# Loading k and v over all 128 partitions, and keeping attention's output in SBUF until its stores

## The chip, the cores and the metric

One core of one Trainium2 chip runs the whole program. The time is device microseconds of one execution. The profile is one further execution, recorded by the hardware profiler; its span is counted from the first to the last instruction of the program.

## The reference

Three stages follow one another. The first is an attention with 32 memory slots for each of 64 heads, the second a dense layer with a sigmoid gate, the third a layer of eight experts with one expert for each token.

```
q, k, v: (8, 8, 576, 64)   phi: (8, 8, 576, 32)
a    = softmax(phi, over the 32 slots)
k_m  = a^T k ;  v_m = a^T v                     # per head: 32 x 64
x    = softmax(q k_m^T / 8) v_m                 # per head: 576 x 64
x    -> (4608 tokens, 512)
h    = x @ w_in (512 x 2048) ; x2 = (h * sigmoid(1.702 h)) @ w_out (2048 x 512)
out  = gate * relu(x2 @ w1[e]) @ w2[e]          # e = the token's best of 8 experts
```

## The kernel before

**Attention.** The 64 heads are worked in 16 groups of four (`NG` = 16, numbered 0 to 15). For a group, SP loads phi (288 KB, `load_phi`), k and v (576 KB each) and q (576 KB, both in `load_qkv`) into one of two buffers, so the loads of group g+2 are issued when group g has released its buffer: `s_phT` for phi, `s_kv` for k and v, `s_qtr` for q. All of these DMAs stand in SP's queue in that order. k takes two DMAs, and so does v: one for heads 0 and 1 on partitions 0 to 63, one for heads 2 and 3 on partitions 64 to 127. The source of each is written with its 64 rows first and the two heads second.

On the compute side VectorE turns phi round (`phi_in`, L1101 and L1103), ScalarE takes its exponential, TensorE transposes it (L619), sums k and v (L631), transposes q (L605) and computes the scores (L649). VectorE does most of the softmax of the group before (L1113 to L1138), and the output matmuls of the group before that are in `out_half` (L590). Each engine goes through its steps in one fixed order. `groups` writes groups 0 to 2 out, runs groups 3 to 14 as three rounds of a loop over four groups, and writes group 15 out.

ScalarE copies the output of a group from PSUM to `xo` (`x_out`, L884), which has two buffers, and stores the group at once (L887) into the DRAM tensor `xT_dram`, on ScalarE's own DMA queue.

**Dense layer.** It runs over nine tiles of 512 tokens. The x of a tile is loaded from `xT_dram` (`load_x`); the first tile needs the tokens of groups 0 and 1 only, the second those of groups 0 to 3. The first load of x is the last but two of SP's DMAs before the tiles. `x_hi` and `x_lo` split x in two float32r parts on ScalarE and VectorE inside the last group, and TensorE starts tile 0 with `mm1(0, 0)` (L672) between the last steps of attention. `mm1` and `mm2` (L706) alternate from there, sixteen of each in a tile, 12 matmuls each.

**Weights.** `W` holds w_in in its first half and w_out in its second, each value as a high and a low part. The first four chunks of w_in are loaded during groups 0 to 3. The other 28 are loaded by SP (`load_w`) and split by GpSimd (`split_w`, L1515 and L1517; `split_w_in`, L1525 and L1527) during tile 0, beginning when the x of tile 0 has been split. `mm1(0, f)` for f = 4, 8, 12 and every `mm2(0, f)` wait for those splits. `stage_a_done` is a wait for all stores of x; it stands on ScalarE and VectorE in step 2 of tile 0 and on SP behind the last load of weights.

**Experts.** The last stage starts from tables that the earlier tiles build; its block loop is not touched. Two constants, `blk8` and `load8`, are loaded between the dense layer and the experts (L527), each from one row of DRAM to one partition.

Of the kernel before, what the change touches and what calls it, by code (L numbers as in the profile page):

```python
# [31 lines left out]
P = 128  # L32
B, H, S, D, M = 8, 8, 576, 64, 32
HG = 4
# [57 lines left out]
def build(nc, q, k, v, phi, w_in, w_out, w_gate, w_ogate, w1, w2, cst, out):  # L92
# [15 lines left out]
    with ExitStack() as ctx:  # L108
# [5 lines left out]

        SLOT = 4 * EW
# [4 lines left out]
        sb("to_512", [P, 96 - RING * (NE + 4)])  # L120
        W = sb("W", [P, 2 * SLOT], F32R)
# [16 lines left out]
        with ExitStack() as a:  # L138
# [25 lines left out]
            xo = sbt(a, "xo", [P, 2, 2, S])  # L164
# [86 lines left out]
        s_xst = [sem(f"xT_stored{i}") for i in range(2)]  # L251
# [63 lines left out]

        def stage_a_done(eng):

            for i in range(2):
                eng.wait_ge(s_xst[i], 16 * B)
# [32 lines left out]
        def groups(eng, body):  # L352
# [3 lines left out]
            with eng.Fori(0, (NG - 4) // 4) as m:  # L356
                for j in range(4):
                    body(4 * m + (3 + j), 2 * m + (3 + j) // 2, (3 + j) % 4)
            body(NG - 1, B - 1, 3)
# [49 lines left out]
        def _(sp):  # L409
# [10 lines left out]
            def load_qkv(g, b, u):  # L420

                wait(sp, s_kv, g - 1)
                for w, src in enumerate((k_v, v_v)):
                    for hh in range(2):
                        heads = src[bass.ds(g * HG + 2 * hh, 2)].rearrange("h (p c) d -> p h (c d)", c=CA)
                        sp.dma_start(kvm[u][hh * PA:(hh + 1) * PA, w], heads).then_inc(s_kvl[u], 16)  # L426
# [42 lines left out]
            with sp.Fori(0, (NG - 8) // 4) as m:  # L469
                for j in range(4):  # L470
                    sp_group(4 * m + (3 + j), 2 * m + (3 + j) // 2, (3 + j) % 4)
            for g in range(NG - 5, NG - 2):
                sp_group(g, g // 2, g % 4)

            for i in range(2):
                sp.wait_ge(s_xst[i], 16)
            load_x(0)
# [19 lines left out]
            def sp_tile(t, first=False, last=False):  # L497
# [3 lines left out]
                if first:  # L501
                    for k in range(1, 4):
# [5 lines left out]
                        if k == 1:  # L508
                            load_x(t + 1)
# [336 lines left out]
        def _(act):  # L846
# [32 lines left out]
            def x_out(g, b, u, i, bank=4):  # L879
# [17 lines left out]
            def group(g, b, r):  # L897
# [14 lines left out]
                if not isinstance(g, int) or g >= 2:  # L912
                    x_out(g - 2, b - 1, u, 0)
# [4 lines left out]
                if not isinstance(g, int) or g >= 2:  # L918
                    x_out(g - 2, b - 1, u, 1)
# [3 lines left out]
            x_out(NG - 2, B - 1, 0, 0)  # L923
# [720 lines left out]
```

## Time and profile before

| what | value |
|---|---|
| median of 3 runs | 1402.93 us (1402.65 to 1410.83) |
| profiled execution, its own time | 1402.57 us |
| its span | 1400.9 us |
| attention, up to the first `mm1` | 153.1 us |
| TensorE busy, whole span | 1351.8 us (96%) |
| TensorE busy, 60 to 80 us | 16.94 of 20 us |
| TensorE busy, 180 to 200 us | 20.00 of 20 us |

The profiled execution's time and its span differ by 1.7 us, which lie around the span. Where the engines are busy all the time a stage is bound by them; where one waits, the row of its wait names what came last. The DMA share is the mean busy share of the 16 DMA engines; it can be over 1, since packets overlap.

### The profile page before, as it was taken

The numbers are of one execution on the slowest core, as the hardware profiler recorded it, in microseconds if no ns is written. First come the engines' busy times: TensorE is split into PE (matmuls) and PEld (weight loads), VectorE is DVE, ScalarE is ACT, GpSimd is POOL, SyncE is SP. The second block draws the span as 40 slices with busy tenths as digits, with TensorE's granted clock in tenths as the row PEclk, the third lists the DMA queues.
The fourth block names the chain that finished last, engine by engine and source line by source line (L and its number), as shares of the span: only waits on it lengthen the run. The fifth ranks groups of instructions, "written<-read, shape, count | busy, mean of one in ns | idle before, by whom it ended". The sixth has DMA issues, their size and how long they took to land.

```text
span 1400.9 us, 26210 instructions
## 1 busy us (share of the span) xinstructions
PE 1351.8 (96%) x7922; PEld 1094.9 (78%) x7923; DVE 681.5 (49%) x1400; ACT 403.2 (29%) x725; POOL 517.7 (37%) x612
## 2 busy tenths in 40 slices
PE   5888899999999999999999999999999999999997
PEld 4566688888888888888888888887788888888885
DVE  4789633344353343433534344436655555555553
ACT  2455422222232232222322223223332222223221
POOL 1100486345443343433433334331434333433331
PEclk9999999999999999999999999999999999999999
DMA  9999635656556556465465654665784688649882
GB/s 229 290 325 313 234 100 168 194 200 194 181 191 183 179 169 182 171 187 175 160 183 176 179 192 147 184 189 203 236 257 119 164 254 249 185 115 261 246 237 61
DMA packets 164843, 275.31 MB, mean 197 GB/s; under 512 B 20179, under 2 KB 57316, under 8 KB 164788
## 3 DMA queue, kind: packets, MB, share of 16 engines
q1 hardware_dynamic: 104260, 197.16, 44.7%
q10 hardware_dynamic: 47408, 45.63, 12.7%
q0 software_dynamic: 13120, 31.82, 7.3%
q8 instruction: 31, 0.51, 0.2%
q14 instruction: 24, 0.20, 0.0%
HBM read 146.03 MB, written 100.45 MB: 176 GB/s over the span
## 4 chain that ended last, share of the span: by engine, by line
PE 86%; DVE 5%; DMA 3%; issue 3%; SPq 2%; ACT 0%; ACTq 0%; POOL 0%; DVEq 0%; POOLq 0%
PE ps L672 28%; PE ps L706 28%; PE ps L776 14%; PE ps L747 14%; DMA ph<-in_phi 1%; PE ps L716 1%; DMA qraw<-in_q 1%; SPq L426 1%; SPq L454 1%; PE ps L649 1%; DVE cmeta L1123 1%; DVE phT L1101 1%; DMA cq<-ch 1%; PE ps L631 0%; DMA cmeta<-record_scratch 0%
## 5 line engine op out<-in xcount | busy, mean ns | idle before, releaser
L672 PE MATMUL ps<-xs,W 128*128 (+1 forms) x1728 | 417.6, 391 | 1.1 <-DVE xs L1162 1.1
L706 PE MATMUL ps<-W,gs 128*128 128x512 f32 x1728 | 415.3, 390 | 0.1
L672 PEld LDWEIGHTS ps<-xs,W 128*128 128x128 f32 x1728 | 323.1, 188 | 72.0 <-issue 4.1
L706 PEld LDWEIGHTS ps<-W,gs 128*128 128x128 f32 x1728 | 324.3, 188 | 68.1 <-DVE gs L1217 0.8
L1215 DVE TENSOR_TENSOR gate<-ps,gate 128x512 f32<-128x512 f32 x144 | 99.6, 691 | 364.0 <-ACT gate L932 363.7
L932 ACT ACTIVATE gate<-ps 128x512 f32<-128x512 f32 x144 | 86.2, 598 | 471.3 <-PE ps L672 470.8
L776 PE MATMUL ps<-W,chT 128*128 (+1 forms) x936 | 218.3, 390 | 1.2 <-DVE chT L1348 1.2
L747 PE MATMUL ps<-W,cx 128*128 (+1 forms) x936 | 218.5, 390 | 0.5 <-issue 0.5
L1540 POOL CAST whi<-raw 128x512 fp32r<-128x512 f32 x128 | 81.3, 635 | 337.9 <-DMA raw<-in_moe_w 337.9
L776 PEld LDWEIGHTS ps<-W,chT 128*128 128x128 f32 x936 | 175.6, 188 | 38.3 <-issue 2.0
L747 PEld LDWEIGHTS ps<-W,cx 128*128 128x128 f32 x936 | 175.6, 188 | 37.3 <-issue 1.1
L1542 POOL TENSOR_TENSOR raw<-raw,whi 128x512 f32<-128x512 f32 x128 | 172.3, 1346 | 21.5 <-POOL whi L1540 20.0
L1217 DVE TENSOR_TENSOR gs<-gate,gs 128x512 fp32r<-128x512 f32 x144 | 120.4, 836 | 99.0 <-ACT gs L936 99.0
L340 POOL DMA_DIRECT2D crec<-record_scratch x160 | 90.0, 562 | 192.1 <-DMA out<-cy,cmeta 114.6
L936 ACT CAST gs<-gate 128x512 fp32r<-128x512 f32 x144 | 89.4, 621 | 115.1 <-DVE gate L1215 113.2
L997 ACT CAST chT<-cqT 128x512 fp32r<-128x512 f32 x41 | 25.2, 620 | 201.4 <-issue 159.8
L1348 DVE TENSOR_TENSOR chT<-cqT,chT 128x512 fp32r<-128x512 f32 x78 | 53.1, 691 | 38.9 <-ACT chT L997 37.6
L1312 DVE TENSOR_TENSOR cx<-cxT,cx 128x512 fp32r<-128x512 f32 x40 | 43.7, 1092 | 57.4 <-ACT cx L965 57.4
L1548 POOL DMA_INDIRECT record_scratch<-rec,posi x36 | 36.3, 1008 | 94.1 <-DVE posi L1277 85.7
L1597 POOL DMA_INDIRECT out<-cy,cmeta x39 | 43.1, 1106 | 70.5 <-ACT cy L1005 62.8
L1326 DVE TENSOR_SCALAR ch<-ps 128x512 f32<-128x512 f32 x37 | 25.5, 691 | 66.5 <-PE ps L747 66.3
L1335 DVE STREAM_TRANSPOSE cqT<-cq 128x512 f32<-128x512 f32 x78 | 50.6, 687 | 13.2 <-DMA cq<-ch 11.4
(158 smaller groups left out, 891.1 us busy)
## 6 DMA issues: line engine op xcount, KB each, us to landing
W<-expert_scratch SPq DMA_DIRECT2D x24, 2048.0 KB, 11.7
raw<-in_moe_w SPq DMA_DIRECT2D x128, 256.0 KB, 2.8
expert_scratch<-whi SPq DMA_DIRECT2D x128, 256.0 KB, 2.6
expert_scratch<-raw SPq DMA_DIRECT2D x128, 256.0 KB, 2.9
cq<-ch ACTq DMA_DIRECT2D x156, 128.0 KB, 3.9
crec<-record_scratch POOLq DMA_DIRECT2D x160, 64.0 KB, 5.6
kvm<-in_k SPq DMA_DIRECT2D x32, 288.0 KB, 5.2
kvm<-in_v SPq DMA_DIRECT2D x32, 288.0 KB, 7.0
```

The costliest lines, as they stand in the source:

```text
L340: eng.dma_start(crec[b * M:(b + 1) * M, r % 3], rows[:, b * P:(b + 1) * P].rearrange("(h n) d -> n h d", n=M)).then_inc(loaded, 16)
L672: mm = pe.matmul(ps[:, f % 2, :], W[:, col:col + P], xs[:, bass.ds(x0 + (x_lo * K1 + c) * T, T)], start=(c == 0 and w_lo + x_lo == 0), sto ...
L706: mm = pe.matmul(ps[:, 2 + s, :], gs[:, f % 2, g_lo, s * P:(s + 1) * P], W[:, col:col + DM], start=(f == 0 and g_lo + w_lo == 0), stop=(f ...
L747: mm = pe.matmul(ps[:, 3 * u + j, :], cx[:, u, x_lo, c, :], W[:, bass.ds(col, 512)], start=(c == 0 and x_lo + w_lo == 0), stop=(c == K1 - ...
L776: mm = pe.matmul(ps[:, 5 + r % 2, :], chT[:, r % 2, h_lo, c, :], W[:, bass.ds(col, DM)], start=(c == 0 and h_lo + w_lo == 0), stop=(c == C ...
L932: act.activation(gate[:, f % 2, :], ps[:, f % 2, :], ACT.Sigmoid, scale=QTOK).then_inc(b_sig, 1)
L936: act.copy(gs[:, f % 2, 0, :], gate[:, f % 2, :]).then_inc(b_ghi, 1)
L1215: dve.tensor_tensor(gate[:, f % 2, :], ps[:, f % 2, :], gate[:, f % 2, :], ALU.mult).then_inc(b_g, 1)
L1217: dve.tensor_tensor(gs[:, f % 2, 1, :], gate[:, f % 2, :], gs[:, f % 2, 0, :].bitcast(F32), ALU.subtract).then_inc(b_glo, 1)
L1348: dve.tensor_tensor(by_h(1, j), cqT[:, j * 512:(j + 1) * 512].rearrange("p (h c n) -> p h c n", h=2, n=M), by_h(0, j).bitcast(F32), ALU.su ...
L1540: pool.tensor_copy(whi[:, u, :], raw[:, u, :]).then_inc(e_hi, 1)
L1542: pool.tensor_tensor(raw[:, u, :], raw[:, u, :], whi[:, u, :].bitcast(F32), ALU.subtract).then_inc(e_lo, 1)
```

## The change

The change has two parts. First, the two DMAs for k (and the two for v) are cut the other way: each covers all 128 partitions and one head of each pair, and its source is written with the pair (2) first and the 64 rows second. Each still moves 288 KB in 128 runs of 2304 bytes.

Second, the copied output of every group stays in SBUF, in `xk`, a region that lies under the part of `W` that the later chunks of weights are split into. The stores are issued in five sets, by different engines: groups 0 and 1 by SP before the loads of group 13, with a wait for them and the first load of x before the loads of group 15; groups 8 and 7 by SP behind all loads; groups 6 and 5 by ScalarE in group 14, groups 4, 3 and 2 in group 15; groups 13, 12, 14, 15 in step 1 of tile 0, and 11, 10, 9 in step 2. GpSimd waits for the stores whose place in `W` it is about to write. The loop over groups now runs twice, and groups 11 to 15 are written out. The wait for all stores moves to ScalarE's step 15 of tile 0 and is gone from VectorE.

```diff
+        STORES = ((0, 1), (8, 7), (6, 5, 4, 3, 2), (13, 12, 14, 15), (11, 10, 9))
...
+            sbt(a, "before_xk", [P, SLOT // 2])
+            xk = sbt(a, "xk", [P, NG * 2 * S])
         W = sb("W", [P, 2 * SLOT], F32R)
...
-            xo = sbt(a, "xo", [P, 2, 2, S])
...
+        def kept(g):
+            return xk[:, bass.ds((NG - 1 - g) * 2 * S, 2 * S)].rearrange("p (a n) -> p a n", a=2)
+        def store_x(eng, i, groups):
+            for g in groups:
+                eng.dma_start(xT_dram[2 * (g % 2) * P:(2 * (g % 2) + 2) * P, g // 2 * S:(g // 2 + 1) * S].rearrange("(a p) n -> p a n", a=2),
+                              kept(g)).then_inc(s_xst[i], 16)
+        def stored_x(eng, i):
+            eng.wait_ge(s_xst[i], 16 * len(STORES[i]))
...
-            with eng.Fori(0, (NG - 4) // 4) as m:
+            with eng.Fori(0, (NG - 8) // 4) as m:
...
-            body(NG - 1, B - 1, 3)
+            for g in range(NG - 5, NG):
+                body(g, g // 2, g % 4)
...
                 for w, src in enumerate((k_v, v_v)):
-                    for hh in range(2):
-                        heads = src[bass.ds(g * HG + 2 * hh, 2)].rearrange("h (p c) d -> p h (c d)", c=CA)
-                        sp.dma_start(kvm[u][hh * PA:(hh + 1) * PA, w], heads).then_inc(s_kvl[u], 16)
+                    heads = src[bass.ds(g * HG, HG)].rearrange("(a h) (p c) d -> h a p (c d)", a=2, c=CA)
+                    for h2 in range(2):
+                        sp.dma_start(kvm[u][:, w, h2], heads[h2]).then_inc(s_kvl[u], 16)
...
+            sp.wait_ge(s_xo, 2 * 2)
+            store_x(sp, 0, STORES[0])
             for g in range(NG - 5, NG - 2):
                 sp_group(g, g // 2, g % 4)
-            for i in range(2):
-                sp.wait_ge(s_xst[i], 16)
-            load_x(0)
+                if g == NG - 4:
+                    stored_x(sp, 0)
+                    load_x(0)
+            sp.wait_ge(s_xo, 2 * 9)
+            store_x(sp, 1, STORES[1])
             load_w(K1, w_out_v[0])
...
                         if k == 1:
+                            stored_x(sp, 2)
                             load_x(t + 1)
...
-                if i == 0:
-                    wait(act, s_xst[u], 16 * b)
-                act.copy(xo[:, u, :, i * HS:(i + 1) * HS], ps[:, bank:bank + 2, 0:HS]).then_inc(s_xo, 1)
-                if i == 1:
-                    wait(act, s_xo, 2 * g + 2)
-                    act.dma_start(xT_dram[2 * u * P:(2 * u + 2) * P, bass.ds(b * S, S)].rearrange("(a p) n -> p a n", a=2),
-                                  xo[:, u]).then_inc(s_xst[u], 16)
+                act.copy(kept(g)[:, :, i * HS:(i + 1) * HS], ps[:, bank:bank + 2, 0:HS]).then_inc(s_xo, 1)
...
+                if isinstance(g, int) and g == NG - 2:
+                    act.wait_ge(s_xo, 2 * 7)
+                    store_x(act, 2, STORES[2][:2])
+                if last:
+                    store_x(act, 2, STORES[2][2:])
...
+                    if first and f == 1:
+                        act.wait_ge(s_xo, 2 * NG)
+                        store_x(act, 3, STORES[3])
                     if first and f == 2:
+                        store_x(act, 4, STORES[4])
+                    if first and f == STEPS - 1:
                         stage_a_done(act)
...
-                    if first and f == 2:
-                        stage_a_done(dve)
...
+                            if f in (0, 4):
+                                stored_x(pool, 1 if f == 0 else 2)
+                            if f == 0:
+                                stored_x(pool, 0)
                             split_w(K1 + 2 * f, 0, SLOT + f * CH)
+                            if k > 1 and c == 0:
+                                stored_x(pool, k + 1)
                             split_w_in(K1 + 2 * f + 1, c, k)
```

## Rows read from the trace of the kernel before

**Rows 1.** The page: the engines' busy time, and the queue that fetches instructions.

```profile
PE 1351.8 (96%) x7922; PEld 1094.9 (78%) x7923; DVE 681.5 (49%) x1400; ACT 403.2 (29%) x725; POOL 517.7 (37%) x612
...
q8 instruction: 31, 0.51, 0.2%
```

**Rows 2.** Stretches of 20 us: PE, PEld, DVE, ACT, POOL, PEclk, DMA share, GB/s.

```profile
120.00:140.00 20.00, 18.00 (x381) 12.92 (x376) 18.58 (x39) 11.86 (x21) 0.00 (x0) 1.00 1.05 301
...
180.00:200.00 20.00, 20.00 (x90) 16.58 (x89) 6.77 (x8) 4.50 (x8) 16.40 (x17) 1.00 0.37 106
```

**Rows 3.** The DMA view of 120 to 130 us, 40 slices of 0.25 us.

```profile
GB/s 230 249 267 286 212 240 230 258 277 258 258 258 221 295 396 424 406 369 387 424 415 406 406 406 424 406 406 378 286 194 258 212 286 240 212 230 249 249 240 221
...
q10 hardware_dynamic: 272, 0.59, 15.0%
```

**Rows 4.** SP's timeline: the DMAs of one group's loads, and of early ones.

```profile
10.93 5.96 SPq L454 DMA_DIRECT2D wg<-in_moe_w_gate  x4
...
21.62 0.43 SPq L418 DMA_DIRECT2D ph<-in_phi  x1
...
123.42 1.25 SPq L426 DMA_DIRECT2D kvm<-in_k  x2
...
126.02 0.59 SPq L429 DMA_DIRECT2D qraw<-in_q  x1
```

**Rows 5.** The waits of 0 to 150 us: total us, times, longest.

```profile
DVE phT L1101 <- DMA ph<-in_phi: 16.9, 8, 4.8
...
PE ps L605 <- DMA qraw<-in_q: 6.5, 4, 4.0
```

**Rows 6.** TensorE's timeline: q of group 0, and the scores of groups 1, 8 and 14.

```profile
12.68 1.12 PE L605 MATMUL ps<-ident,qraw 128*128 128x128 f32 x4 [4.00 <-DMA qraw<-in_q]
...
29.48 1.22 PE L649 MATMUL ps<-qT,kmT 64*32 64x288 f32 x16 [0.65 <-DVE kmT L1184]
...
94.41 0.72 PE L649 MATMUL ps<-qT,kmT 64*32 64x288 f32 x16 [0.39 <-DVE kmT L1184]
...
142.41 0.72 PE L649 MATMUL ps<-qT,kmT 64*32 64x288 f32 x16 [0.40 <-DVE kmT L1184]
```

**Rows 7.** VectorE's timeline: phi of group 2.

```profile
24.96 0.78 DVE L1101 STREAM_TRANSPOSE phT<-ph 128x576 f32<-128x576 f32 x1 [2.90 <-DMA ph<-in_phi]
```

**Rows 8.** The DMA view of 917.7 to 919.7 us, around `blk8` and `load8`.

```profile
q1 hardware_dynamic: 4, 0.00, 0.3%
...
raw<-const_blk SPq DMA_DIRECT2D x1, 1.3 KB
```

**Rows 9.** TensorE's timeline from the last group's q to the first `mm1`.

```profile
144.25 0.66 PE L605 MATMUL ps<-ident,qraw 128*128 128x128 f32 x4
...
148.63 0.41 PE L631 MATMUL ps<-kvm,am 64*32 64x128 f32 x6 [1.35 <-issue]
...
153.13 3.02 PE L672 MATMUL ps<-xs,W 128*128 128x512 f32 x12 [1.08 <-DVE xs L1162]
```

**Rows 10.** Stretches of 4 us, columns as in the second group.

```profile
24.00:28.00 4.00, 0.42 (x4) 0.18 (x2) 2.86 (x8) 1.44 (x3) 0.00 (x0) 0.85 1.05 258
28.00:32.00 4.00, 2.99 (x43) 1.78 (x45) 3.28 (x8) 0.03 (x1) 0.00 (x0) 0.50 1.03 318
```

**Rows 11.** Timelines in tile 0: VectorE's end of step 2, split 11, `mm2(0, 2)`, `mm1(0, 4)`.

```profile
169.45 1.26 DVE L1217 TENSOR_TENSOR gs<-gate,gs 128x512 fp32r<-128x512 f32 x1 [0.80 <-ACT gs L936]
...
171.26 1.29 POOL L1527 TENSOR_TENSOR W<-raw,W 128x512 fp32r<-128x512 f32 x1
...
173.98 2.88 PE L706 MATMUL ps<-W,gs 128*128 128x512 f32 x12
176.70 2.88 PE L672 MATMUL ps<-xs,W 128*128 128x512 f32 x12
```

**Rows 12.** ScalarE's timeline: the copy that follows the store issued in group 15.

```profile
156.88 0.64 ACT L884 COPY xo<-ps 128x576 f32<-128x576 f32 x1 [4.15 <-PE ps L590]
```

**Rows 13.** The DMA view of 146 to 148 us: the queue that fetches instructions.

```profile
q8 instruction: 1, 0.02, 3.0%
```

More of the change, by code:

```diff
@@ L120, in build @@
         sb("to_512", [P, 96 - RING * (NE + 4)])
+        with ExitStack() as a:
+            sbt(a, "before_xk", [P, SLOT // 2])
+            xk = sbt(a, "xk", [P, NG * 2 * S])
         W = sb("W", [P, 2 * SLOT], F32R)
@@ L250, in build @@
         s_xo = sem("attn_out_copied")
-        s_xst = [sem(f"xT_stored{i}") for i in range(2)]
+        s_xst = [sem(f"xT_stored{i}") for i in range(len(STORES))]
         s_passed = {e.engine: sem(n) for e, n in ((nc.vector, "vector_waits_passed"), (nc.gpsimd, "pool_waits_passed"),
@@ L314, in build @@
         block = ctx.enter_context(nc.Block())
+        def kept(g):
[6 more added lines that the diff above has]
+            eng.wait_ge(s_xst[i], 16 * len(STORES[i]))
         def stage_a_done(eng):
-            for i in range(2):
-                eng.wait_ge(s_xst[i], 16 * B)
+            for i in range(len(STORES)):
+                stored_x(eng, i)
         STEPS = C1
@@ L471, in _ @@
                     sp_group(4 * m + (3 + j), 2 * m + (3 + j) // 2, (3 + j) % 4)
+            sp.wait_ge(s_xo, 2 * 2)
+            store_x(sp, 0, STORES[0])
             for g in range(NG - 5, NG - 2):
                 sp_group(g, g // 2, g % 4)
-            for i in range(2):
-                sp.wait_ge(s_xst[i], 16)
-            load_x(0)
+                if g == NG - 4:
[3 more added lines that the diff above has]
+            store_x(sp, 1, STORES[1])
             load_w(K1, w_out_v[0])
@@ L877, in q_out, with x_out @@
                     act.copy(q_flat[:, 512:QA * D], ps[:, 2:4, :].rearrange("p k n -> p (k n)")[:, 512 - P:]).then_inc(s_qT, 1)
-            def x_out(g, b, u, i, bank=4):
+            def x_out(g, i, bank=4):
                 wait(act, s_o, 2 * g + i + 1)
-                if i == 0:
-                    wait(act, s_xst[u], 16 * b)
-                act.copy(xo[:, u, :, i * HS:(i + 1) * HS], ps[:, bank:bank + 2, 0:HS]).then_inc(s_xo, 1)
-                if i == 1:
-                    wait(act, s_xo, 2 * g + 2)
-                    act.dma_start(xT_dram[2 * u * P:(2 * u + 2) * P, bass.ds(b * S, S)].rearrange("(a p) n -> p a n", a=2),
-                                  xo[:, u]).then_inc(s_xst[u], 16)
+                act.copy(kept(g)[:, :, i * HS:(i + 1) * HS], ps[:, bank:bank + 2, 0:HS]).then_inc(s_xo, 1)
             def x_hi(t, c):
@@ L912, in group @@
                 if not isinstance(g, int) or g >= 2:
-                    x_out(g - 2, b - 1, u, 0)
+                    x_out(g - 2, 0)
                 q_out(g, 1)
@@ L918, in group @@
                 if not isinstance(g, int) or g >= 2:
-                    x_out(g - 2, b - 1, u, 1)
+                    x_out(g - 2, 1)
+                if isinstance(g, int) and g == NG - 2:
[3 more added lines that the diff above has]
+                    store_x(act, 2, STORES[2][2:])
             exp_phi(0, 0)
             groups(act, group)
-            x_out(NG - 2, B - 1, 0, 0)
+            x_out(NG - 2, 0)
             exp_scores(NG - 1)
-            x_out(NG - 2, B - 1, 0, 1, 2)
+            x_out(NG - 2, 1, 2)
             def g_step(t, f):
@@ L1034, in _ @@
             g_step(0, 0)
-            x_out(NG - 1, B - 1, 1, 0, 6)
-            x_out(NG - 1, B - 1, 1, 1)
+            x_out(NG - 1, 0, 6)
+            x_out(NG - 1, 1)
             tiles(act, act_tile)
```

## Prediction

> **What bounds the kernel now.** I read the page first. TensorE is busy 96% of the span [rows 1], so time can be had only where it is not. The view by stretches finds that place: from 180 us on TensorE is busy 20.00 of 20 us, between 120 and 140 us 18.00 [rows 2]. Attention ends where `mm1(0, 0)` starts, at 153.13 us [rows 9]; everything after it, 1247.8 us, is matmuls back to back, and the change touches only its first 70 us.
>
> Inside attention the view of waits comes next. VectorE waited for phi 8 times, 16.9 us in all, and TensorE for q 4 times, 6.5 us [rows 5]. TensorE's timeline says when: group 1's scores start at 29.48 us, group 8's at 94.41, group 14's at 142.41 [rows 6]. That is 9.3 us for each of the first seven groups and 8.0 us for each of the next six. The 8.0 us is the engines' own: VectorE is busy 18.58 of 20 us there [rows 2]. So the early groups are bound by loads.
>
> The DMA view says what the loads do. The 16 engines are occupied in every slice, yet the rate has two levels: some 210 to 290 GB/s while a group's k and v, issued from 123.42 us on, go to half of the partitions, and 369 to 424 GB/s while its q and x move [rows 3, 4].
>
> **The k and v loads.** Per group 1.18 MB go at about 240 GB/s (4.9 us) where q's rate of about 400 would take 2.9 us. If the new DMAs run at q's rate, all loads of a group take 2.06 MB / 400 = 5.2 us, well inside 8.0 us.
>
> But the new source has two rows in its outer index, where every large DMA of the kernel has at least 32 on both sides. What shares a DMA out over the engines? Two kinds of row speak to it. A store of x (256 runs) leaves 272 packets, 256 and one closing packet for each of 16 engines [rows 3]. The loads of `blk8` and `load8`, one row each, left 4 packets together [rows 8]: one run and one closing packet each, so one engine each. A DMA of one row is thus not cut up. It is the rows that are handed out. Two rows on one side then can be handed to two engines, 64 runs each. No row of the trace shows a large DMA of this kind, so I bound it.
>
> At best it is spread over 16 engines, as above. If it goes to two, each carries half of 294,912 B. One engine's rate at the upper level is 416 / 16 = 26 GB/s [rows 3]; 147,456 B take 5.67 us. One engine alone, fetching instructions, shows a lower rate: 0.51 MB in 31 transfers is 16.5 KB [rows 1], and its 3.0% of 16 engines for 2 us is 0.96 us [rows 13], so 17 GB/s. The packets of the first row are of the kind in question, so I take 26 and keep 17 for the far end. Then, on the two busiest engines:
> - k and v: 16 groups x 4 DMAs x 5.67 us = 363 us.
> - q and phi: 16 x (36,864 + 18,432) B / 26 GB/s = 34 us.
> - Four chunks of w_in, the constants, the stores of groups 0 and 1 and the first x tile, now all ahead of group 15's q: 0.21 MB, 8 us.
>
> Together 405 us. With 2.3 us before the first k is issued and 2 us to land, the last q is there at about 409.5 us. The loads stay queued without a gap, since two buffers are kept and a group's 8 us of work hide under 25 us of loads. From the last q to `mm1(0, 0)` the kernel takes 153.13 - 144.25 = 8.9 us [rows 9]. TensorE will by then have waited some 17 us in each group. After its 4 us wait for phi the granted clock was 0.50, the lower level of 1.2 GHz, in the next 4 us [rows 10], so I add 3 us. `mm1(0, 0)` starts at 421.4 us, 268 us later than now. Of the profiled time that makes 1402.6 + 268 = 1671 us; the median of the runs is 0.4 us above the profiled time, which I leave out. I say 1670.
>
> The Trainium skill has a rule for this ("DMA: Bandwidth & Descriptors", "Why a DMA increments its semaphore by 16 and not by 1"): the number of engines is the largest one up to 16 that divides the slowest dimension, not of size 1, on both sides. By it the new loads (2 and 128) run on two engines. The row of the one-row DMAs agrees; no row of this trace shows a two-row one. The same skill ("SBUF — State Buffer", "Door 1: The DMA port swizzle") says that partitions 0 to 63 reach 8 of 16 ports, which is why the change looks attractive, and the two rates above agree.
>
> **The stores.** Fourteen of 16 leave the load phase. Each was 0.59 MB, 1.5 us of all engines. In the forecast most of this is free, as 14 engines idle. If the loads are spread, it takes each group's traffic from 2.65 to 2.06 MB. ScalarE issues two stores instead of one in group 14 and three in group 15, at about 0.4 us; in group 15 it next waits 4.15 us [rows 12], which hides them. In tile 0 it issues four and three. `g_step(0, 2)` stands behind the four, 1.6 us; it ends now at 170.71 us and `mm2(0, 2)` takes its result at 173.98 [rows 11], 3.3 us of room.
>
> **The waits.** SP's wait for the stores of groups 0 and 1 has the first x load and group 15's loads queued behind it; the stores were issued a group earlier, so it costs nothing. GpSimd's waits are the risk: 4.1 MB of stores share the rings with the weight chunks in tile 0. Split 11 ends at 172.55 and `mm1(0, 4)`, which needs it, starts at 176.70 [rows 11], 4.1 us of room against a delay I bound at 0 and 8 us: below by idle rings, above by eight chunks each 1 us late. That costs 0 to 4 us; I take 0.
>
> **Five groups written out.** Their code has to be fetched. In group 15, the one written out now, TensorE stood 1.35 us inside the sum of k and v [rows 9]. Four more such stops cost 0 (hidden under loads) to 5.4 us. In the forecast they are hidden.
>
> **Rival 1, the loads are spread over 16 engines: faster.** For it: nothing in the source forces one engine to walk one row. Against it: the one-row DMAs. Price: k and v of group 0 save 2.0 us ahead of its q, which lands now just before 12.68 us [rows 6]. VectorE then waits 2.90 us for phi of group 2, which is issued at 21.62 us behind eight small loads; the first four took 5.96 us to issue where two of k's take 1.25 [rows 4, 7]. At k's pace the four take 2.5 us, 3.5 less, the eight some 6.8 less. So group 1 gains 2.0 to 6.8 us; I take 5.4, since the queue would have drained before most of them. Groups 1 to 8 then go at 8.0 us: 64.9 - 56.0 = 8.9 us. Together 14.3 us, less 2 us for stops and late weights: 1390 us, from 1385 to 1397. It decides as soon as the new loads reach about 300 GB/s.
>
> **Rival 2, spread, but given back.** The early groups gain as in rival 1, and the stores in tile 0 hold up the weights by 4 us, the code costs 5.4 us and the slow issues stay: 14.3 - 4 - 5.4 - 3.4 = 1.5 us, so 1401 us, from 1397 to 1410.
>
> **Rival 3, two engines at the lower rate.** 10.54 MB / 17 GB/s = 620 us instead of 405: 1886 us, and anything from 1700 between.
>
> **How the numbers follow.** The forecast has 0.64, from 1640 (two engines alone may run somewhat above 26 GB/s: 29 GB/s takes 42 us off, to 1629; half of that is inside) to 1700. Rival 1 has 0.25, rival 2 has 0.06, rival 3 0.05. The two main cases lie far apart and both are needed to hold 0.8, so the range is 1385 to 1700; the forecast's own range is 1640 to 1700. A measurement of this kernel can tell about 1% from no change, 14 us. Rival 1 lies around that bound, 1388.9 us: 0.10 of it is below and 0.15 above. Faster 0.10, same 0.15 + 0.06 = 0.21, slower 0.69.
>
> **What would show it.** In the profile of the changed kernel: times from issue to landing of k and v of 20 us or more, a DMA share of 0.15 to 0.25 and about 80 GB/s (2.06 MB in 25 us) through attention, waits of TensorE for q or k of 15 us in each group, scores 25 us apart. A closing-packet count of 2 for each load would show the cause itself. If rival 1 holds, scores are 8.0 us apart from group 1 on, the rate reaches 400 GB/s while k and v move, and VectorE's waits for phi fall from 16.9 to a few us. My forecast is wrong if the engines are given out by the destination's rows alone. The stores would show in GpSimd's waits before the split of chunk 12 and in a gap of TensorE before `mm1(0, 4)` or `mm1(0, 8)`.

## The result, and the profile after

The changed kernel takes 1692.8 us (1691.9 to 1693.9, 4 runs) beside 1406.9 us for the kernel before (1402.7 to 1413.6, 4 runs): ratio 1.203, interval 1.197 to 1.209. The profiled execution took 1693.2 us with a span of 1691.4. The first `mm1` starts at 437.47 us, before at 153.13 [rows 9]: 284.3 us later. From there to the end the span has 1253.9 us, before 1247.8. So by the two profiled executions 284 of 290 us went into attention, 6 behind it.

The page of the changed kernel (busy time, the span in 40 slices, and the chain that ended last):

```profile
span 1691.4 us, 26106 instructions
...
PE 1379.7 (82%) x7922; PEld 1115.4 (66%) x7923; DVE 675.2 (40%) x1400; ACT 404.9 (24%) x725; POOL 519.6 (31%) x612
...
PE   2243342342799999999999999999999999999997
...
PEclk9575666766899999999999999999999999999999
DMA  2322212324636656564646464655648739765892
...
PE 70%; SPq 24%; DMA 3%; POOL 1%; issue 1%; DVE 0%; ACTq 0%; ACT 0%; DVEq 0%; POOLq 0%
```

TensorE's 96% [rows 1] has become 82%. The first ten slices (423 us) hold the loss: TensorE is busy 2 to 4 tenths of each slice, the DMA engines 1 to 4 tenths, 2.3 on average. An engine that waits for data while the DMA engines are mostly idle: that is the pattern to learn here. The chain names SP's queue with 24% of the span, some 400 us, which is nearly all of attention. Its loads were issued late because issuing them was itself slow, as SP's timeline shows for two groups (us, duration, then the DMA issued):

```profile
101.96 8.35 SPq L449 DMA_DIRECT2D kvm<-in_k  x2
110.36 11.22 SPq L449 DMA_DIRECT2D kvm<-in_v  x2
121.62 6.10 SPq L452 DMA_DIRECT2D qraw<-in_q  x1
127.76 0.58 SPq L457 DMA_DIRECT2D raw<-in_moe_w_in  x1
128.75 0.35 SPq L440 DMA_DIRECT2D ph<-in_phi  x1
129.30 8.04 SPq L449 DMA_DIRECT2D kvm<-in_k  x2
137.45 11.15 SPq L449 DMA_DIRECT2D kvm<-in_v  x2
```

k's pair was issued in 1.25 us before [rows 4]; v's now takes 11.2 us, 5.6 for each DMA. That is what one DMA takes on two engines: 147,456 B at 26 GB/s are 5.67 us. I read it so: the queue is full, and each issue waits for one DMA to drain.

The DMA view of 140 to 150 us, while SP issues one v and begins with q, in 40 slices of 0.25 us:

```profile
DMA  1111111111111111111111111111114111111111
GB/s 55 55 55 46 46 55 55 55 46 46 55 55 55 46 46 55 55 55 46 46 55 55 46 46 55 55 55 46 46 55 121 55 46 46 55 55 55 46 46 55
DMA packets 228, 0.53 MB, mean 53 GB/s; under 512 B 3, under 2 KB 3, under 8 KB 227
```

A flat 53 GB/s, where half-partition loads gave 210 to 290 [rows 3]; one or two tenths of 16 engines. And the small packets: 3 in 10 us, in which 0.53 MB or 1.8 DMAs of 288 KB went. Two closing packets for each DMA make 3.6; sixteen would make 29. A whole group's loads, in the same view of 109 to 136 us, count out exactly:

```profile
DMA packets 962, 2.38 MB, mean 88 GB/s; under 512 B 56, under 2 KB 56, under 8 KB 959
```

56 small packets are 16 each for q, phi and a chunk of w_in, and 2 for each of the four DMAs of k and v. Two engines, then.

The waits of TensorE and VectorE from 0 to 440 us (total us, times, longest), which answer to [rows 5]:

```profile
PE ps L634 <- DMA qraw<-in_q: 280.5, 16, 22.0
...
DVE phT L1135 <- DMA ph<-in_phi: 265.2, 16, 21.8
```

q is waited for in each of 16 groups, 17.5 us on average; it has no fault of its own and only stands behind k and v. The scores of groups 0, 1, 14 and 15 start at 36.68, 64.82, 405.51 and 435.67 us: 26.6 us for each group, on average, where [rows 6] have 8.0 to 9.3.

TensorE's timeline at the end of attention and in tile 0, and its clock in stretches of 4 us (PE, PEld, DVE, ACT, POOL, PEclk, DMA share, GB/s):

```profile
428.25 1.12 PE L634 MATMUL ps<-ident,qraw 128*128 128x128 f32 x4 [20.83 <-DMA qraw<-in_q]
...
435.67 0.72 PE L678 MATMUL ps<-qT,kmT 64*32 64x288 f32 x16
...
437.47 3.01 PE L701 MATMUL ps<-xs,W 128*128 128x512 f32 x12 [1.08 <-DVE xs L1196]
...
461.74 2.98 PE L701 MATMUL ps<-xs,W 128*128 128x512 f32 x12 [1.28 <-POOL W L1559]
...
487.20 4.58 PE L701 MATMUL ps<-xs,W 128*128 128x512 f32 x12 [3.42 <-POOL W L1559]
```

```profile
424.00:428.00 4.00, 0.00 (x0) 0.00 (x0) 0.00 (x0) 0.00 (x0) 0.00 (x0) 0.50 0.36 131
428.00:432.00 4.00, 3.75 (x56) 3.13 (x60) 0.00 (x0) 1.62 (x3) 0.00 (x0) 0.50 0.13 46
432.00:436.00 4.00, 3.97 (x58) 2.33 (x50) 2.46 (x6) 1.76 (x4) 0.00 (x0) 0.81 0.00 0
```

After 20.8 us without work the clock is granted at 0.50 (1.2 GHz) up to 432 us. Yet the path from the last q to `mm1(0, 0)` takes 437.47 - 428.25 = 9.2 us, against 8.9 [rows 9].

The 6 us behind the first `mm1` are in tile 0, where TensorE now waits twice for GpSimd's splits. The 100 us after the first `mm1`, of the changed kernel and of the one before:

```profile
437.47:537.47 100.00, 94.50 (x411) 76.32 (x412) 35.65 (x48) 26.83 (x44) 69.36 (x71) 0.98 0.54 183
```

```profile
153.13:253.13 100.00, 98.46 (x438) 80.44 (x439) 40.69 (x52) 29.13 (x48) 73.22 (x75) 1.00 0.50 158
```

27 matmuls fewer, which at 98.46 / 438 = 0.225 us make 6.1 us. TensorE is idle for 5.5 us instead of 1.5, 4.0 us more. The other 2.1 us are slower matmuls. Most of them are the twelve that start at 487.20 us, behind the wait of 3.42: they take 4.58 us, where those of 461.74 take 2.98, and the granted clock from 488 to 492 us is 0.57. That GpSimd was late for want of data is in its own timeline:

```profile
466.57 0.61 POOL L1547 CAST W<-raw 128x512 fp32r<-128x512 f32 x1 [4.97 <-DMA raw<-in_moe_w_out]
```

ScalarE issues the stores of seven groups ahead of that, four at 448.91 us and three at 453.95, and SP the x of the next tile (1 MB) at 454.28. The chunk, issued at 458.81 us behind them, took 7.6 us to land, where the median of these chunks is 2.7. That it queued behind the stores is my reading; no run takes the stores alone out of the changed kernel's tile 0.

### The profile page after: what moved, and what is told of

Read it like the earlier page. It is cut to its first block, busy times and chain, and to the rows that moved or that the text cites. A ratio compares the mean times of both kernels' runs of the same rounds, so it can differ in the third digit from the quotient of the medians.

```text
span 1691.4 us, 26106 instructions
## 1 busy us (share of the span) xinstructions
PE 1379.7 (82%) x7922; PEld 1115.4 (66%) x7923; DVE 675.2 (40%) x1400; ACT 404.9 (24%) x725; POOL 519.6 (31%) x612
## 4 chain that ended last, share of the span: by engine, by line
PE 70%; SPq 24%; DMA 3%; POOL 1%; issue 1%; DVE 0%; ACTq 0%; ACT 0%; DVEq 0%; POOLq 0%
PE ps L701 22%; PE ps L735 22%; SPq L449 17%; PE ps L805 12%; PE ps L776 12%; SPq L452 5%; DMA raw<-in_moe_w_out 2%; SPq L440 1%; DMA qraw<-in_q 1%; PE ps L745 1%; POOL W L1549 1%; SPq L477 1%; ACTq L1019 0%; POOL W L1547 0%; PE ps L660 0%
## 5 line engine op out<-in xcount | busy, mean ns | idle before, releaser
L634 PE MATMUL ps<-ident,qraw 128*128 128x128 f32 x144 | 30.2, 351 | 280.5 <-DMA qraw<-in_q 280.5
L634 PEld LDWEIGHTS ps<-ident,qraw 128*128 128x128 f32 x144 | 20.0, 175 | 289.2 <-DMA qraw<-in_q 248.3
L1251 DVE TENSOR_TENSOR gs<-gate,gs 128x512 fp32r<-128x512 f32 x144 | 115.5, 802 | 98.9 <-ACT gs L965 98.9
L1135 DVE STREAM_TRANSPOSE phT<-ph 128x576 f32<-128x576 f32 x16 | 12.5, 778 | 265.2 <-DMA ph<-in_phi 265.2
L1547 POOL CAST W<-raw 128x512 fp32r<-128x512 f32 x16 | 11.0, 689 | 313.3 <-DVE xs L1196 295.8
L904 ACT COPY qT<-ps 128x512 f32<-128x512 f32 x16 | 9.4, 586 | 266.5 <-PE ps L634 266.5
```

Of the source, the lines that this page charges most:

```text
L1251: dve.tensor_tensor(gs[:, f % 2, 1, :], gate[:, f % 2, :], gs[:, f % 2, 0, :].bitcast(F32), ALU.subtract).then_inc(b_glo, 1)
```

## The experiments

The theory: a DMA is handed out to the engines by the rows of its outermost dimension, on both sides, so the new loads use two engines. Its rivals: loads over all partitions are slow in themselves, whatever the source; or the stores and the written-out groups carry a large part. The first four runs separate the change's parts.

**e1_kv_alone**: the kernel before, with the new k and v loads and nothing else.

```diff
-                    for hh in range(2):
-                        heads = src[bass.ds(g * HG + 2 * hh, 2)].rearrange("h (p c) d -> p h (c d)", c=CA)
-                        sp.dma_start(kvm[u][hh * PA:(hh + 1) * PA, w], heads).then_inc(s_kvl[u], 16)
+                    heads = src[bass.ds(g * HG, HG)].rearrange("(a h) (p c) d -> h a p (c d)", a=2, c=CA)
+                    for h2 in range(2):
...
+                        sp.dma_start(kvm[u][:, w, h2], heads[h2]).then_inc(s_kvl[u], 16)
```

> The kernel before with only the new k and v loads; x is stored at once as before. My theory (a load with two outer source rows runs on two engines): the stores of x add their sixteenth, 14 x 36,864 B / 26 GB/s = 20 us, to the same two engines, and tile 0 loses its 6 us of late weights, so 1692.8 + 20 - 6 = about 1707 us (1690 to 1720), with q landing some 27 us apart. Rival (the late stores and their waits hold up the loads): close to the kernel before, 1395 to 1415 us.

Measured: 1702.0 us (2 runs), ratio 1.208 (1.203 to 1.214); the first `mm1` at 446.87 us. The loads alone do all the damage. The first `mm1` is even 9.4 us later than in the changed kernel, since here 14 more stores of 0.59 MB run among the loads; 20 us were expected. The 9.4 us are the difference of the seven groups from 5 to 12 alone: their scores come 26.8 us apart here and 25.4 in the changed kernel, so a store costs 1.35 us there, near the 1.4 us that a sixteenth of it (36,864 B) takes at 26 GB/s. Before and behind these groups the two kernels' differences cancel.

**e2_stores_alone**: the changed kernel with the old k and v loads, so the other half of the change.

> The changed kernel with the old k and v loads; x is kept and stored late. My theory: no group waits longer than before; k and v take 4.9 us and q and phi 2.2 us of a group's 8.0, so the early groups gain up to 9 us, and tile 0 gives back some 5 to 6 us through late weights: 1399 us (1394 to 1405). Rival (late stores carry the loss): above 1600 us. Rival 2 (nothing is gained early): 1408 to 1413 us.

Measured: 1416.2 us (7 runs), ratio 1.0076 (1.0040 to 1.0113): slower, where a small gain was expected. The DMA view of 40 to 80 us, and two waits of 0 to 156 us:

```profile
GB/s 351 404 236 253 235 260 239 256 267 380 295 206 230 212 270 253 240 270 285 188 249 224 242 260 244 260 258 111 44 212 260 256 247 247 267 371 242 311 249 235
```

```profile
DVE phT L1134 <- DMA ph<-in_phi: 14.8, 8, 5.7
...
PE ps L659 <- issue: 7.0, 10, 3.2
```

Taking the stores out of this phase brought nothing: the scores of group 10 start at 110.22 us, before at 110.33, and phi is still waited for 14.8 us (16.9 in [rows 5]). The half-partition loads, at some 240 GB/s, still bind. Then come the costs: groups 11 to 15 are written out, and from the scores of group 10 to those of group 15 it is 44.4 us, before 41.0; tile 0 has a wait of 3.2 us for GpSimd; and the experts one of 4.0 us for a transposed input, where the longest of the kernel before is 0.7. I found no cause for the last.

**e3_adjacent_late, e4_adjacent_early**: loads over all 128 partitions whose source is 128 rows in one dimension. The two heads of one DMA are neighbours in DRAM, so head and row fold into one index. Since a pair of heads then lies the other way round on the partitions, the transposes of `a` pick their columns so as to match, and the sum of k and v swaps its indices; neither adds an instruction. e3 has it in the changed kernel, e4 in the kernel before.

```diff
+                    for h2 in range(2):
+                        heads = src[bass.ds(g * HG + 2 * h2, 2)].rearrange("h (p c) d -> (h p) (c d)", c=CA)
+                        sp.dma_start(kvm[u][:, w, h2], heads).then_inc(s_kvl[u], 16)
...
-                        tr = pe.matmul(ps[rows, c // 8, (c % 8) * 2 * M:(c % 8 + 1) * 2 * M], aT[rows, c * PA:(c + 1) * PA],
-                                       ident[rows, rows], start=True, stop=True, tile_position=(hh * PA, hh * PA))
+                        pick = ident[:].rearrange("p (b a m) -> p a b m", b=2, a=2)[:, hh]
+                        tr = pe.matmul(ps[rows, c // 8, (c % 8) * 2 * M:(c % 8 + 1) * 2 * M], aT[:, c * PA:(c + 1) * PA],
+                                       pick, start=True, stop=True, tile_position=(0, hh * PA))
...
-                        hh, h2 = h // 2, h % 2
+                        h2, hh = h // 2, h % 2
```

> The changed kernel, but with the two heads of one load next to each other in DRAM, so that its source is 128 rows in one dimension; the transposes of a pick the heads to match. Same partitions, bytes and run length as the changed kernel. My theory: 16 engines, k and v at some 400 GB/s, groups 8.0 us apart from group 1 on, tile 0 still late by 5 to 6 us: 1393 us (1387 to 1399). Rival (a load over all 128 partitions is itself slow): above 1600 us.

> The kernel before with the adjacent-head loads of the last run and nothing else: x is stored at once. My theory: 2.65 MB in each group at some 400 GB/s take 6.6 us of 8.0, so the stores need not be late, and tile 0 has no gap: 1389 us (1385 to 1394), faster than the version with late stores. Rival (the stores still crowd the loads): 1396 to 1403 us, with the late version ahead.

Measured: e3 1403.8 us (12 runs), ratio 0.9959 (0.9935 to 0.9983), first `mm1` at 147.75 us. e4 1392.6 us (6 runs), ratio 0.9893 (0.9862 to 0.9923), first `mm1` at 141.22 us. Loads over all 128 partitions are thus fast, and the first rival falls; the second fell with e1. The same 2304-byte runs, the same bytes, the same partitions: what differs from the changed kernel is the shape of the source, and with it which head lies where. The DMA view of e4, 40 to 80 us, and its wait for phi:

```profile
GB/s 399 418 382 399 410 394 394 387 372 247 294 242 198 304 290 297 348 399 396 350 306 270 214 359 390 383 364 357 325 325 293 283 399 394 346 258 327 336 233 286
```

```profile
DVE phT L1102 <- DMA ph<-in_phi: 4.1, 3, 1.9
```

The plateaus at 240 GB/s are gone and the waits for phi fall from 16.9 to 4.1 us. From group 2 on the scores come 8.1 us apart on average. This is what the change was after, and it comes without the stores. e3 against e4, the same loads with and without the moved stores, has intervals that don't touch: the rest of the change costs about 0.7%, 10 us.

**e5_written_out**: e4 with five groups written out instead of one, the stores as before.

```diff
-            with eng.Fori(0, (NG - 4) // 4) as m:
+            with eng.Fori(0, (NG - 8) // 4) as m:
...
-            body(NG - 1, B - 1, 3)
+            for g in range(NG - 5, NG):
+                body(g, g // 2, g % 4)
```

> The kernel of e4 (adjacent heads, stores at once) with one more edit: the loop over groups runs twice and groups 11 to 15 are written out, as in the changed kernel. In e3 groups 10 to 15 took 45.1 us where e4 takes 39.7. My theory: that is the fetch of code that is written out, with TensorE standing in L631 and L619 for want of instructions, so this run is 4 to 6 us above e4, at some 1397 us. Rival (the stalls of e3 come from the stores and their waits): as e4, within 1.5 us.

Measured: 1402.2 us (12 runs), ratio 0.9972 (0.9946 to 0.9998). By the medians that is 9.6 us above e4, by the ratios 11, and the first `mm1` is 10.8 us later, twice what was expected; with e4's gain this is nearly all given back. TensorE's timeline in e5, where the first written-out group begins, then the same place in e4:

```profile
99.83 0.72 PE L651 MATMUL ps<-qT,kmT 64*32 64x288 f32 x16 [0.40 <-DVE kmT L1186]
102.58 2.12 PE L633 MATMUL ps<-kvm,am 64*32 64x128 f32 x66 [0.24 <-ACT am L866]
107.71 0.41 PE L633 MATMUL ps<-kvm,am 64*32 64x128 f32 x6 [3.01 <-issue]
111.13 1.21 PE L651 MATMUL ps<-qT,kmT 64*32 64x288 f32 x16
...
118.43 0.85 PE L633 MATMUL ps<-kvm,am 64*32 64x128 f32 x22 [2.26 <-issue]
...
129.53 2.31 PE L633 MATMUL ps<-kvm,am 64*32 64x128 f32 x39 [2.67 <-issue]
```

```profile
99.71 0.72 PE L650 MATMUL ps<-qT,kmT 64*32 64x288 f32 x16 [0.40 <-DVE kmT L1185]
...
102.61 2.17 PE L632 MATMUL ps<-kvm,am 64*32 64x128 f32 x72 [0.26 <-issue]
...
107.87 0.72 PE L650 MATMUL ps<-qT,kmT 64*32 64x288 f32 x16 [0.39 <-DVE kmT L1185]
```

Up to 102.6 us the two are alike. Then the 72 matmuls of one sum, one group in e4, break into 66 and 6, with 3.01 us between in which TensorE waits for nothing that the profile shows. Three such stops, of 3.01, 2.26 and 2.67 us, stand in three of the written-out groups; inside the loop no stop of this line is above 0.3 us. The scores of groups 10 to 15 start at 99.83, 111.13, 122.97, 134.62, 142.45 and 150.18 us: three groups of 11.3 to 11.8 us where a looped one takes 8.0, and then two of 7.8, without a stop. The three carry all of the 10.8 us, and the stops in this line 7.9 of them. From 99 to 120 us the queue that fetches instructions moved two blocks in e5 and none in e4:

```profile
q8 instruction: 2, 0.03, 0.6%
```

The times fit as well: each of the three stops, viewed by itself, has one such block, and from 99 us to the last stop no block falls between them. But one block between 129.53 and 135 us and two between 142 and 150 us come without a stop. So the stops go with the fetch of code; why only some fetches are waited for is open.

Nor is 10.8 us a fixed price. From the scores of group 10 to those of group 15, e4 takes 39.7 us and e5 50.4, but e3, with the same groups written out and the stores moved, takes 45.1: its stops are of 3.29, 1.23 and 1.20 us. So in attention the moved stores do save something beside written-out groups: e3's first `mm1` is 4.2 us ahead of e5's (one profiled execution of each). It is lost again behind it: tile 0 has 428 matmuls in its first 100 us where e5 has 438 (2.2 us), and the waits for `chT` in the experts are 5.8 us instead of 1.8. The intervals of e3 and e5 overlap.

**e6_tile_stores_early**: e3 with eight stores drawn forward, the seven of tile 0 and group 8's; SP issues them in its loop rounds. They carry the x of group 1, the same number of bytes.

```diff
-                        store_x(act, 3, STORES[3])
-                        store_x(act, 4, STORES[4])
...
+                    sp.wait_ge(s_xo, 2 * 2)
+                    half_of = j % 2
+                    sp.dma_start(xT_dram[2 * half_of * P:(2 * half_of + 2) * P, bass.ds((2 * m + 4 + j // 2) * S, S)].rearrange("(a p) n -> p a n", a=2),
+                                 kept(1)).then_inc(s_early, 16)
```

> The kernel of e3 (adjacent heads, late stores), but the seven stores of tile 0 and that of group 8 are issued by SP one at a time in the two loop rounds, with group 1's x in place of their own (so eight groups get wrong data). Nothing is stored in tile 0. My theory: the seven stores crowd the weight chunks, so the gap of TensorE before the later matmuls of tile 0 goes and the run is 5 to 6 us under e3, about 1398 us; attention is as in e3. Rival (tile 0 is late for another reason, such as code or the x load): as e3, 1404 us.

Measured: 1396.3 us (10 runs), ratio 0.9925 (0.9902 to 0.9948). By the medians it is 7.5 us below e3, but the kernel before was 3.8 us faster beside it; by the ratios it is about 5 us. The interval overlaps e3's by a little, so a gain is likely and not shown beyond doubt. The 100 us after the first `mm1`, of e3 and of e6:

```profile
147.75:247.75 100.00, 97.89 (x428) 79.52 (x429) 38.31 (x50) 28.59 (x47) 69.47 (x73) 0.98 0.55 187
```

```profile
146.43:246.43 100.00, 99.14 (x441) 80.92 (x442) 41.16 (x52) 29.12 (x48) 71.97 (x75) 1.00 0.48 155
```

Without the stores of seven groups the traffic is 155 instead of 187 GB/s and 13 more matmuls fit in, 2.9 us. But e3 has no wait for GpSimd here. It waits 2.11 us for VectorE's `pT` where e6 waits 0.86, and behind that wait its granted clock is 0.80 and 0.78 in two stretches of 4 us, from 155 to 163 us: 1.3 us of waiting and 1.7 us of slower matmuls, the whole 2.9 us. On average its clock is 0.98, where e6 has 1.00; e4, whose tile 0 has none of these stores, has 0.98 and 429 matmuls too. So these two rows don't charge the stores with anything; what does is the wait for GpSimd in e2 and in the changed kernel, 3.2 and 4.7 us. Why e3 has none is open. Another 3.5 us of e3's loss to e6 lie in the experts, in the waits for `chT` (5.8 us against 2.3).

**e7_gates_later**: e4, with the ten small loads of gate weights moved from ahead of group 2's loads to behind those of groups 3 and 4, five behind each (`sp_group(g)` issues the loads of group g + 2).

```diff
+            def load_gates(i):
...
             for g in range(3):
                 sp_group(g, g // 2, g)
+                if g:
+                    load_gates(g - 1)
```

> The kernel of e4, with the ten small loads of the gate weights moved behind the loads of groups 3 and 4 in SP's queue. In e4 group 2's phi is issued at 17.68 us behind them and groups 2 and 3 are 9.3 and 8.5 us apart from the ones before. My theory: those go to 8.0 us, 1 to 2 us under e4, about 1391 us. Rival (the small loads delay group 5's loads as much): as e4.

Measured: 1390.5 us (6 runs), ratio 0.9882 (0.9848 to 0.9916), first `mm1` at 138.31 us. It is the fastest of all, 2.0 us below e4 by the medians, 1.5 by the ratios and 2.9 by the first `mm1`; the intervals of the two overlap, so over the whole kernel the gain isn't shown. The scores start at 16.60, 24.27 and 31.96 us, where e4 had 17.11, 25.29 and 34.59.

**e8_four_rows, e9_eight_rows**: the changed kernel with more outer rows in the source of k and v, at the same bytes for a group. e8 has four rows of 32 runs of 4608 bytes in a DMA of 576 KB; e9 eight rows of 16 runs of 9216 bytes in one DMA of 1152 KB for the whole group, all of it from k. The first two added lines are e8's, the other three e9's.

```diff
+                    heads = src.rearrange("(a h) (p c) d -> h a p (c d)", h=2, c=18)[0][bass.ds(g, 4)]
+                    sp.dma_start(kvm[u][:, w].rearrange("p h n -> p (h n)"), heads).then_inc(s_kvl[u], 32)
...
+                    if w == 0:
+                        heads = src.rearrange("(a h) (p c) d -> h a p (c d)", h=2, c=36)[0][bass.ds(g, 8)]
+                        sp.dma_start(kvm[u][:].rearrange("p w h n -> p (w h n)"), heads).then_inc(s_kvl[u], 64)
```

> The changed kernel with k and v loaded by one DMA each, from four rows (every second head) of 32 runs of 4608 bytes: wrong heads, the same bytes for the same 128 partitions. My theory (the outer source rows are handed to engines): four engines, 589,824 B / 4 / 26 GB/s = 5.67 us for each of two DMAs, 11.3 us in a group beside some 3.4 us for q and phi, so groups 14 to 15.5 us apart and 1500 to 1525 us. Rival (two engines whatever the count): as the changed kernel, 1690 us. Rival (any full set of partitions with a split source is equally slow by its run length): between them.

> The changed kernel with k and v replaced by one DMA of 1152 KB from eight rows (every second head) of 16 runs of 9216 bytes, k's data only: wrong data, the same bytes and partitions. My theory: eight engines, 1,179,648 B / 8 / 26 GB/s = 5.67 us in a group, beside 3.4 us for q and phi, so 9.1 us, groups just over 9 us apart and some 1415 to 1430 us. Rival (four engines at most for a split source): as e8, 1517 us.

Measured: e8 1517.3 us (one run), first `mm1` at 261.80 us, as expected. e9 1493.5 us (one run), far off the expected 1415 to 1430, first `mm1` at 225.60 us. The DMA views of 100 to 120 us, slices of 0.5 us, e8 and then e9:

```profile
GB/s 111 189 318 438 341 180 244 217 83 111 111 101 101 111 101 101 111 111 101 101 127 175 230 332 378 175 153 74 101 101 97 115 101 124 217 304 157 92 111 101
```

```profile
GB/s 111 88 88 60 41 60 18 28 157 60 235 147 175 147 313 240 138 184 97 189 194 176 97 147 111 147 230 138 267 157 175 134 171 226 272 217 210 235 124 65
```

e8 has the flat plateau at 101 to 111 GB/s, four times 26, and peaks of 300 to 438 in the stretches of q and phi. e9 has no plateau. Three things had changed at once in it, the rows, the length of the runs and the size of the DMA, so the next pair changes the rows alone.

**e10_eight_rows_short, e11_sixteen_rows**: the changed kernel, its four DMAs of 288 KB and its runs of 2304 bytes, with 8 rows of 16 runs and 16 rows of 8 runs. The edit shown is e10's; e11 has `bass.ds(g, 16), 0:8`.

```diff
-                    heads = src[bass.ds(g * HG, HG)].rearrange("(a h) (p c) d -> h a p (c d)", a=2, c=CA)
+                    heads = src.rearrange("(a h) (p c) d -> h a p (c d)", h=2, c=CA)[0][bass.ds(g, 8), 0:16]
...
-                        sp.dma_start(kvm[u][:, w, h2], heads[h2]).then_inc(s_kvl[u], 16)
+                        sp.dma_start(kvm[u][:, w, h2], heads).then_inc(s_kvl[u], 16)
```

> The changed kernel with its own four k and v loads a group (128 runs of 2304 bytes over all partitions), but from eight outer source rows (every second head) of 16 runs: wrong data. e9 gave 1493.5 us where eight engines at 26 GB/s would give 1415 to 1430. Theory A (e9's long runs of 9216 bytes slow an engine down): eight engines at 26 GB/s here, 5.7 us for k and v in a group, 1415 to 1430 us. Theory B (with eight engines another limit comes first, such as where their writes or reads meet): as e9, 1480 to 1500 us.

> As e10, from sixteen outer source rows of 8 runs of 2304 bytes. Sixteen engines by the rule that rows are handed out. If a split source costs nothing else, as e3: groups 8.0 us apart and some 1404 us. If B holds for e10, then 1420 to 1450 us here, with k and v under 300 GB/s; two engines would give 1690 us.

Measured: e10 1424.6 us, first `mm1` at 180.35 us; e11 1398.5 us, first `mm1` at 149.68 us (one run each). e10 lies inside the range that was expected, e11 5.5 us below it. The DMA view of 100 to 120 us of e10 and of 60 to 80 us of e11:

```profile
GB/s 180 138 198 207 207 203 207 207 217 184 217 230 198 300 290 290 226 272 240 157 184 203 203 217 207 207 207 198 212 198 244 318 295 295 230 263 221 157 203 203
```

```profile
GB/s 263 263 304 309 336 143 166 180 359 304 258 198 226 267 304 341 281 318 281 290 263 115 143 189 300 134 203 355 309 217 286 258 286 276 332 332 336 263 42 46
```

The plateau is at 207 GB/s for eight rows, and gone for sixteen. In order, with all else as in the changed kernel (but e3's heads lie the other way round, and e8 has runs twice as long; e8 to e11 read other heads of k and v than the computation wants, in part the same ones in neighbouring groups, which shifts how the tokens fall on the experts, and they have one run each; so the first `mm1` is the column to read):

| outer rows of the source | rate while k and v move | first `mm1` | time |
|---|---|---|---|
| 2 | 53 GB/s | 437.5 us | 1692.8 us |
| 4 (e8) | 101 to 111 GB/s | 261.8 us | 1517.3 us |
| 8 (e10) | 207 GB/s | 180.4 us | 1424.6 us |
| 16 (e11) | no plateau | 149.7 us | 1398.5 us |
| 128 (e3) | no plateau | 147.8 us | 1403.8 us |

That is 26 GB/s for each row up to eight. Per group, k and v take 1.18 MB / 53 = 22.3, / 105 = 11.2 and / 207 = 5.7 us; the first differences, 11.1 and 5.5 us, times 16 groups make 178 and 88 us, and the first `mm1` moved by 175.7 and 81.4.

With the rows so accounted for, e9 shows what the rest of its edit does: with the same eight rows it is 45.3 us later than e10 at the first `mm1`, 2.8 us in each group. Whether it is the length of the runs or the size of the DMA (1152 KB) that costs, no run here separates.

## Why the prediction was right or wrong

The direction and the mechanism were right, and 1670 us was 23 us too low; 1692.8 lies inside the range and inside the forecast's own 1640 to 1700. In the profiled execution the last q was 18.7 us later than in the sum, the path behind it 2.7 us shorter (9.2 instead of 8.9 + 3), and tile 0 lost 6.1 us where nothing was taken: 22.1 us, from 1671 to 1693.2. So the 3 us for the clock, which were too much, hid a little of the rest.

- **Two engines.** Right: two closing packets for each DMA, a plateau at 53 GB/s, and the ladder from 2 to 16 rows. Rival 1 and rival 2 (spread over 16) and rival 3 (17 GB/s each) are out. "It is the rows that are handed out" was drawn from DMAs of one row [rows 8] and held for 2, 4, 8 and 16. The Trainium skill's rule ("DMA: Bandwidth & Descriptors", "Why a DMA increments its semaphore by 16 and not by 1"), that the number of engines is the largest up to 16 that divides the slowest dimension of both sides, agrees with all these; the destination had 128 rows each time, so the source alone decided.
- **5.67 us for each DMA at 26 GB/s.** Right: SP's issues are 5.6 us apart, 53 GB/s for two engines.
- **q and phi, 34 us, and others, 8 us.** This is the step that was off, in size: the term of the sum for what follows k and v. A group took 26.6 us instead of 25.3, k and v 22.3 to 22.7 of it; so q, phi and the rest take about 3.9 to 4.3 us in place of 2.6 (34 and 8 us over 16 groups). Both parts were too small. From the scores of group 5 to those of group 12 (172.84 to 350.95 us), where next to nothing but k, v, q and phi is loaded, a group takes 25.4 us instead of the sum's 22.7 + 2.1; over 16 groups that is some 10 of the 18.7 us. The rest lies at both ends, where the chunks, the constants, the stores and x are: 26.6 to 28.1 us for each of the first five intervals, 30.2 for the last. In that last one run two stores that the sum had left out, those of groups 6 and 5, which ScalarE issues at 405.46 us: by their bytes 2.8 us on each engine, and v's pair, issued at 394.97, held SP for 16.7 us instead of 11.2. q and phi had been counted as bytes at 26 GB/s on each engine from the moment the two engines are free. Between the k and v of one group and the next the engines ramp up and down: the DMA view of 109 to 136 us has 119, 201, 348, 316, 334, 308, 164 GB/s in seven slices of 0.675 us around q, phi and a chunk, never 416. SP, too, spends 6.1 us on issuing q behind v before it comes to the next loads. Which of the two sets the extra time no run separates. The last q was there at 428.25 us, not at 409.5.
- **3 us for the clock.** The clock was as expected, the cost was not. The sum of k and v, 72 matmuls, took 4.06 us at 0.50, where it took 2.12 and 0.41 us of work and a stop of 1.35 us between [rows 9]. The slow clock cost 1.5 us, and the stop, hidden now under the wait for q, gave 1.35 back: 9.2 us for the path instead of 8.9.
- **Tile 0, taken at 0 (bounds 0 and 4).** 27 matmuls fewer in 100 us, 6.1 us. Two waits for GpSimd make 4.7 of it and the slow clock behind the longer one 1.6, while another wait is 0.7 shorter. It is above the bound: I had looked at the splits of w_in alone, and the chunk that came late was one of w_out, ahead of which GpSimd stood 4.97 us.
- **The written-out groups, hidden (0 to 5.4 us).** In the changed kernel they were hidden, under 17.5 us of waiting in each group. As a price without cover, 5.4 us fits e3 (45.1 us from group 10 to 15, e4 39.7) and is half of what e5 shows, 10.8 us. I had multiplied the 1.35 us of [rows 9] by four; the stops are only three, in e5 of 2.3 to 3.0 us, and a group loses 3.3 to 3.8 us with one.
- **The stores.** "Mostly free" was wrong for the groups that wait on two engines: a store adds its sixteenth to these two as well, 1.35 us in each of the middle groups (e1 against the changed kernel). In the sum that weighs little, but it should have held four stores ahead of the last q and not two. What I left open in rival 1 and 2: over the whole kernel the moved stores gain nothing that the runs can show. With the old loads k and v bind (e2), and with good ones what attention gains is lost again behind it (e3 against e5).
- **Rival 1's price, were the loads spread.** It came close: 14.3 us less 2 for stops gave 1390 us, and e4, with the spread loads alone, took 1392.6. Its first `mm1` comes 11.9 us earlier than before, not 14.3. One reading in it was wrong: the 3.5 us for the first four small loads were nearly doubled to 6.8 for all eight, though the second four took only 4.18 us to issue before; in e4 the eight take 7.3 us instead of 10.1, and group 1's scores come 4.2 us earlier, where 5.4 was taken. With the whole change around them (e3) it is 1403.8, which is rival 2's case, 1401 us from 1397 to 1410. So rival 2 was the better of these two, and I had given it 0.06 against 0.25, for want of the price of straight-line code. These two chances were not tested by the change itself, where the loads were not spread.

## What to carry to other kernels

Before cutting a DMA anew, look at the outermost dimension of its source: with 2, 4 and 8 rows there it used as many engines and left the others idle, though it filled all 128 partitions. Fold the pair of heads and the rows into one dimension, by choosing neighbours, and the same bytes are spread (1692.8 against 1403.8 us). A small outermost dimension of the destination, and numbers of rows that don't divide 16, no run here tried. The tell-tale is a flat rate that is a small multiple of 26 GB/s, two closing packets for each DMA in place of 16, and an issuing queue whose issues take as long as a transfer. And price straight-line code that replaces a loop: here four more written-out groups took back 11 of the 15 us that the better loads gave (e4, e5, by the ratios).

## What the hardware showed that I had not expected

- Issuing isn't free of what it issues: with two engines' queues full, as I read it, each DMA of v held SP for 5.6 us, where it takes 0.6 us otherwise [rows 4], and q, for which 14 engines stood idle, was issued behind it.
- Longer runs in larger DMAs weren't better: eight rows with 16 runs of 9216 bytes gave the first `mm1` at 225.6 us, eight rows with 16 runs of 2304 bytes, four times as many DMAs, at 180.4 us. One run each, and the two aren't separated.
- A stop in a straight-line group took 2.3 to 3.0 us in e5, each with one block of code fetched in it, and 1.2 to 3.3 us in e3, against at most 0.3 us inside the loop.
- A wait of 3.42 us in tile 0 cost more than itself: the granted clock was 0.57 in the 4 us behind it, and twelve matmuls took 4.58 us instead of 2.9 to 3.0.
- Left open: a wait of TensorE for `chT` in the experts, 4.8 us in e2 and 5.8 us in e3, against 1.2 to 1.6 in the kernel before, in e4 and in the changed kernel, and 2.3 in e6. The size goes with no part of the change: e2, e3 and the changed kernel all store late.
